# Weight splitting in an attention and MoE kernel: other tiles for the first layer, other engines for the scaling, the high and the low parts, and another instruction for the row sums

## What is computed

```python
# attention, 8 heads of 64, a window of 128 keys, a distance bias per head
attn = softmax(where(mask, q @ k.T / 8 + bias, -1e9)) @ v          # sum + 1e-9 in the softmax
# first MLP on x = attn (512 features), 2048 hidden
xn = (x - mean) / sqrt(var + 1e-6) * g_ln
x = x + relu(xn @ w_ch1) @ w_ch2
# second MLP, 1024 hidden, gated by a 3-tap convolution along the tokens
h = relu(x @ w_in)
out = (h * sigmoid(conv3(h, conv_w))) @ w_out
```

## Time and profile before

| | us |
|---|---|
| median of 3 runs | 806.03 (805.5 to 806.35) |
| the profiled execution: its own time | 807.84 |
| the profiled execution: span of its instructions | 806.0 |
| PE busy in the span | 783.7 (97%) |
| DVE, ACT, POOL busy | 520.0, 372.3, 171.9 |
| mean granted TensorE clock | 0.998 |

### The profile page before, as it was taken

One profiled execution on the slowest core, in us unless ns is written; L12 is line 12 of the kernel. 1 busy time (PEld: TensorE's weight loads), 2 busy tenths in 40 slices (PEclk: granted clock), 3 DMA queues, 4 the chain that ended last, 5 costly groups with the idle time before them and its releaser, 6 DMA issues.

```text
span 806.0 us, 17023 instructions
## 1 busy us (share of the span) xinstructions
PE 783.7 (97%) x5809; PEld 754.6 (94%) x5809; DVE 520.0 (65%) x1419; ACT 372.3 (46%) x1033; POOL 171.9 (21%) x165
## 2 busy tenths in 40 slices
PE   9989799999999999989999999999999999999998
PEld 5668789999999999989999999999998999999998
DVE  6785777873667776456777646213259888788862
ACT  6884465652346555224655522113244444444532
POOL 5677832210212121011212101111210111011100
PEclk9999999999999999999999999999999999999999
DMA  7653512211221230122123012303230202222001
GB/s 186 172 163 99 185 37 75 71 42 59 68 68 39 74 92 21 59 71 68 39 74 86 27 59 83 106 13 96 80 100 10 82 31 81 81 81 81 22 23 45
DMA packets 56494, 59.42 MB, mean 74 GB/s; under 512 B 25184, under 2 KB 43616, under 8 KB 55904
## 3 DMA queue, kind: packets, MB, share of 16 engines
q1 hardware_dynamic: 56416, 58.43, 24.5%
HBM read 44.25 MB, written 14.16 MB: 72 GB/s over the span
## 4 chain that ended last, share of the span: by engine, by line
PE 74%; issue 11%; DVE 8%; ACT 3%; POOL 3%; POOLq 0%; DVEq 0%; ACTq 0%
PE bank L1378 21%; PE bank L1380 20%; PE bank L1379 20%; PE bank L1317 3%; PE bank L1349 3%; PE bank L1331 3%; PE bank L1276 1%; PE bank L1302 1%; POOL small L684 1%; PE bank L1289 1%; DVE prob L1029 1%; ACT prob L805 1%; DVE small L1022 1%; DVE q_st L1116 1%; PE bank L1265 1%
## 5 line engine op out<-in xcount | busy, mean ns | idle before, releaser
L1378 PE MATMUL bank<-xn_hi,wa_hi 128*128 128x288 f32 x512 | 156.4, 306 | 2.7 <-issue 2.7
L1378 PE MATMUL bank<-h_hi,wb_hi 128*128 128x288 f32 x512 | 156.3, 305 | 1.1 <-DVE h_lo L1086 0.6
L1379 PE MATMUL bank<-xn_lo,wa_hi 128*128 128x288 f32 x512 | 152.1, 297 | 0.0
L1380 PE MATMUL bank<-xn_hi,wa_lo 128*128 128x288 f32 x512 | 151.8, 296 | 0.0
L1379 PE MATMUL bank<-h_lo,wb_hi 128*128 128x288 f32 x512 | 150.9, 295 | 0.0
L1380 PE MATMUL bank<-h_hi,wb_lo 128*128 128x288 f32 x512 | 150.7, 294 | 0.0
L835 ACT ACTIVATE h_hi<-bank 128x288 fp32r<-128x288 f32 x128 | 52.4, 409 | 173.1 <-PE bank L1380 172.2
L1086 DVE SCALAR_TENSOR_TENSOR h_lo<-bank,h_hi 128x288 fp32r<-128x288 f32 x128 | 58.2, 455 | 113.9 <-ACT h_hi L835 112.3
L1378 PEld LDWEIGHTS bank<-xn_hi,wa_hi 128*128 128x128 f32 x512 | 96.7, 189 | 4.2 <-issue 3.4
L1378 PEld LDWEIGHTS bank<-h_hi,wb_hi 128*128 128x128 f32 x512 | 96.5, 189 | 3.3 <-issue 2.0
L1379 PEld LDWEIGHTS bank<-xn_lo,wa_hi 128*128 128x128 f32 x512 | 96.9, 189 | 0.0
(11 more groups left out here) (132 smaller groups left out, 1679.0 us busy)
## 6 DMA issues: line engine op xcount, KB each, us to landing
k_raw<-qkT SPq DMA_DIRECT2D x48, 144.0 KB, 2.9
q_raw<-qkT SPq DMA_DIRECT2D x48, 144.0 KB, 2.9
x_in<-x_spill SPq DMA_DIRECT2D x8, 580.0 KB, 4.3
ch_in<-ch_spill SPq DMA_DIRECT2D x8, 580.0 KB, 5.2
x_spill<-xT SPq DMA_DIRECT2D x4, 1152.0 KB, 4.2
ch_spill<-ch_stage SPq DMA_DIRECT2D x32, 144.0 KB, 1.9
out<-out_stage SPq DMA_DIRECT2D x32, 144.0 KB, 1.8
wa_raw<-w SPq DMA_DIRECT2D x16, 256.0 KB, 3.7
```

Source lines behind the costliest of these rows:

```text
L1378: nc.tensor.matmul(dst, w_h, a_h, start=start, stop=False)
L1379: nc.tensor.matmul(dst, w_h, a_l, start=False, stop=False)
L1380: last = nc.tensor.matmul(dst, w_l, a_h, start=False, stop=stop)
```

## The change

For the first MLP's first layer, a tile is now 128 rows by 512 columns of `w_ch1` as it lies in memory: tile i = 4j + d has rows 128d and columns 512j. So each of its rows has one gain, which ACT takes as `scale` while it rounds, and DVE as the scalar of the one instruction that makes the low part, (raw x gain) - hi. `first_product` f now reads from the four tiles 4(f//4) + d and waits for all four. `w_gain` is gone. All tiles of `w_ch2` are rounded and subtracted on POOL. The times of the tiles are new tables, six of `wa` and nine of `wb` in the prologue. The row sums and the constant 1e-9 lie side by side (`sum_eps`), and a tensor_reduce over the pairs replaces tensor_scalar_add; in the prologue it stands at +1.4 instead of +1.78 slots. In the pass last, the tiles of the second MLP wait for the last of the four blocks that share their columns; the last four (`LATE_W` = 12) come in the second MLP's first section, rounded by ACT and subtracted by POOL.

```diff
+W1_PROLOGUE, W1_FIRST = [2.1, 3.1, 4.1, 5.1, 6.1, 7.1], [0.25, 2.05, 3.85, 5.65, 7.45, 9.25, 11.05, 12.85, 14.65, 16.45]
+W2_PROLOGUE, W2_FIRST = [3.0, 4.5, 6.0, 7.5, 9.0, 10.2, 11.4, 12.6, 13.8], [1.5, 3.9, 6.3, 8.7, 11.1, 13.5, 15.9]
...
+LATE_W = NW2 - DC
+def last_step(m):
+    return m // DC * DC + DC - 1
...
-        out += [(2 * (F1 + m) + 1, ("W", NW1 + m)) for m in range(NW2)]
+        out += [(2 * (F1 + last_step(m)) + 1 + 2 * (m % DC), ("W", NW1 + m)) for m in range(LATE_W)]
...
+                if layer == 1:
+                    j, d = divmod(i, DC)
+                    return w1[P * d:P * (d + 1), DM * j:DM * (j + 1)], wa_hi[:, i, :], wa_lo[:, i, :]
...
+        def w1_part(w, f, d):
+            return w[:, DC * (f // DC) + d, P * (f % DC):P * (f % DC + 1)]
+        def hi_by_pool(n):
+            return n < NW1 and not first_layer(n)
+        def lo_by_pool(n):
+            return not first_layer(n) if n < NW1 else n % 2 == 1 or n >= NW1 + LATE_W
...
-                nc.gpsimd.tensor_tensor(kc, kc, g_col[:].unsqueeze(2).broadcast_to((P, DC, P)), ALU.mult).then_inc(w_prep, 1)
...
+            for m in range(LATE_W, NW2):
+                w_lo(NW1 + m)
...
-                nc.scalar.activation(w_tile(n)[1], w_raw(n), ACT.Copy).then_inc(w_hi_ready, 1)
+                nc.scalar.activation(w_tile(n)[1], w_raw(n), ACT.Copy, scale=gain(n) if first_layer(n) else 1.0).then_inc(w_hi_ready, 1)
...
+                        if first and 1 <= f <= NW2 - LATE_W:
+                            w_hi(NW1 + LATE_W + f - 1)
...
-                nc.vector.tensor_scalar_add(row_inv[:, r:r + n], row_sum[:, r:r + n], SUM_EPS).then_inc(half_sum, 1)
+                nc.vector.tensor_reduce(row_inv[:, r:r + n], sum_eps[:, r:r + n, :], AX, ALU.add).then_inc(half_sum, 1)
...
+                if first_layer(n):
+                    nc.vector.scalar_tensor_tensor(lo, w_raw(n), gain(n), hi.bitcast(F32), ALU.mult, ALU.subtract).then_inc(w_split_dve, 1)
...
-("HS", 1.78, "half_inverse")
+("HS", 1.4, "half_inverse")
...
-                    wait_w_split(pe, 2 * f)
+                    wait_w_split(pe, W_ORDER.index((1, last_step(f))))
...
+            for n in (LATE_W - 2, LATE_W - 1, NW2 - 1):
+                wait_w_split(pe, NW1 + n)
```

More of the change, by code:

```diff
@@ L23 @@
 ACT = mybir.ActivationFunctionType
+AX = mybir.AxisListType.X
 P = 128
@@ L102 @@
 X_SPILL_AT, LOAD_AT = 6.5, -1.9
-W_TIMES = [2.4, 3.6, 4.8, 6.0, 7.2, 8.4, 9.2, 10.0, 10.8, 11.6, 12.4, 13.2, 14.0, 14.8]
-W_PROLOGUE = len(W_TIMES)
-W_HI_POOL = (4, 8, 12)
-W_PACE, W_AHEAD = 1.0, 6
-LEAD_GAIN_PROLOGUE = 0.5
-assert W_PROLOGUE % 2 == 0
+W1_PROLOGUE, W1_FIRST = [2.1, 3.1, 4.1, 5.1, 6.1, 7.1], [0.25, 2.05, 3.85, 5.65, 7.45, 9.25, 11.05, 12.85, 14.65, 16.45]
+W2_PROLOGUE, W2_FIRST = [3.0, 4.5, 6.0, 7.5, 9.0, 10.2, 11.4, 12.6, 13.8], [1.5, 3.9, 6.3, 8.7, 11.1, 13.5, 15.9]
+W_TIMES = sorted([(kind == "first", t, layer) for layer, kind, times in ((1, "prologue", W1_PROLOGUE), (1, "first", W1_FIRST),
+                                                                      (2, "prologue", W2_PROLOGUE), (2, "first", W2_FIRST)) for t in times])
+W_ORDER = [(layer, sum(x[2] == layer for x in W_TIMES[:n])) for n, (_, _, layer) in enumerate(W_TIMES)]
+W_AHEAD = 6
+assert len(W_ORDER) == NW1 and len(set(W_ORDER)) == NW1
 def head_items(start, slots=6.0, frame=FRAME, lag=LAG):
@@ L165, in timeline @@
         out += [(t, ("WARM", n)) for t, n in WARM]
-        out += [(t, ("W", n)) for n, t in enumerate(W_TIMES)]
+        out += [(t, ("W", n)) for n, (first, t, _) in enumerate(W_TIMES) if not first]
         return sorted(out, key=lambda x: x[0])
@@ L169, in timeline @@
     if kind == "first":
-        out += [(0.25 + W_PACE * (n - W_PROLOGUE), ("W", n)) for n in range(W_PROLOGUE, NW1)]
+        out += [(t, ("W", n)) for n, (first, t, _) in enumerate(W_TIMES) if first]
         out += HALF_FIRST
@@ L445, in w_raw @@
             if n < NW1:
-                return (wb_raw if n % 2 else wa_raw)[:, n // 2, :]
+                layer, i = W_ORDER[n]
+                return (wa_raw if layer == 1 else wb_raw)[:, i, :]
             return w_stage[:, n % NSTAGE, :]
@@ L700, in w_hi @@
             def w_hi(n):
-                if n % 2 == 0:
-                    pool.wait_ge(w_prep, n // 2 + 1)
                 wait_w_loaded(pool, n)
@@ L710, in run @@
             def run(kind, batch):
-                lead = LEAD_GAIN_PROLOGUE if kind == "prologue" else 1.5
                 early = 0.7 if kind == "prologue" else 1.0
-                delays = [("PREP", 0.1, "k_lo"), ("PREPV", 0.1, "v_lo"), ("IN", 0.5, "inv"), ("W", -lead, "w_gain"), ("W", 0.0, "w_hi"),
+                delays = [("PREP", 0.1, "k_lo"), ("PREPV", 0.1, "v_lo"), ("IN", 0.5, "inv"), ("W", 0.0, "w_hi"),
                           ("W", 0.3, "w_lo"), ("Y", 1.0, "y"), ("HS", -early, "scale"), ("HS", 0.9, "pads")]
@@ L888, in run @@
                         evacuate(batch, a[0])
-                    elif name == "w" and a[0] not in W_HI_POOL:
+                    elif name == "w" and not hi_by_pool(a[0]):
                         w_hi(*a)
@@ L1021, in normalise @@
                 dve.wait_ge(exp_ready, NT * hd + t1)
-                nc.vector.tensor_scalar_add(row_sum[0:rows, t0:t1], row_sum[0:rows, t0:t1], SUM_EPS).then_inc(sum_step, 1)
+                nc.vector.tensor_reduce(row_inv[0:rows, t0:t1], sum_eps[0:rows, t0:t1, :], AX, ALU.add).then_inc(sum_step, 1)
                 dve.wait_ge(sum_step, step + 1)
-                nc.vector.reciprocal(row_inv[0:rows, t0:t1], row_sum[0:rows, t0:t1]).then_inc(sum_step, 1)
+                nc.vector.reciprocal(row_inv[0:rows, t0:t1], row_inv[0:rows, t0:t1]).then_inc(sum_step, 1)
                 dve.wait_ge(sum_step, step + 2)
@@ L1152, in run @@
                         evacuate(batch, a[0])
-                    elif name == "w" and not by_pool(a[0]):
+                    elif name == "w" and not lo_by_pool(a[0]):
                         w_lo(*a)
```

87 lines of the change are left out of this document (40 added, 47 removed).

## The result

The changed kernel takes 807.04 us (median of 20 runs, 805.96 to 808.67) beside 805.88 for the kernel before on the same chip; the ratio is 1.0014, 95% interval 1.0008 to 1.0020. On another chip it was 807.66 us, 1.0018 (1.0009 to 1.0028). So it makes no difference of note, where 801.3 was forecast with a range up to 806.5. The profiled execution has a span of 806.3 us and took 808.14, 0.3 more than that of before.

A forecast was written before the change was run, and what follows sets the result against it. The prediction took PE as the bound, busy 783.7 of 806.0 us, with 13.5 us within reach of the weight work. Terms of 8.8 us back less 4.1 lost gave 4.7, so 801.3 us, range 796.5 to 806.5.

The forecast's parts named there:

- 10 to 61: Prologue heads and the stretch behind, in us: 0.8 back up to 45, 3.0 back from 45 to 61.
- rival 3: Slower: each low part on DVE waits for a whole POOL operation, making DVE the bound; 815.5 us, chance 0.12.
- 75 to 102: Third power, DVE chain from 90 to 98 and clock after it: 0.8, 2.1 and 1.7 us back.
- the two terms for PE's waits, 0.8 and 2.1: PE idle time won back: 0.8 us from 75 to 90, 2.1 us from 90 to 98.
- The term for the third power: 75 to 90: less weight work on POOL ahead, power 1.1 us sooner; 0.8 us back, bounds 0 and 1.8.
- three low parts ahead of the first transposed probabilities: 90 to 98: three low parts in DVE's list cost 2.1 us, against 3.2 and 1.0 us of waits removed.
- The third term: 98 to 102: PE idles less before it, so the clock stays full; 1.7 us back, bounds 0 and 1.7.
- 102 to 115: Two more low parts cost 2.1 us against 2.5 us of removed waits: 0.4 back, bounds -0.5 and 1.6.
- 115 to 594: No weight work, and later tiles in the pass last run beside a full PE: nothing won or lost.
- The second MLP: From 594: four POOL subtractions each hold DVE 1.0 us, ACT's roundings add 0.1; cost 4.1 us, bounds 0 and 6.9.
- Rival 4: All as forecast, but the clock falls in the second MLP, costing 1.7 us: 803.0 us, chance 0.08.
- Rival 2: The start wins half: power still late, low parts on the path after 84, clock falls; 806.3 us, chance 0.16.

The follow-up runs named there:

- e15: The kernel before with the reduction over pairs alone, half_inverse left at 1.78: 803.68 us, ratio 0.9955 to before.
- "after": Column of relu start times in the changed kernel's first profile, relative to the kernel before (minus is sooner); changed kernel 807.04 us.
- the second profile: The changed kernel run once more, nothing altered, for another profile: 807.66 us.
- e5: The changed kernel with POOL's seven second-layer tiles of the first pass 4.8 time units later, behind the powers: 803.97 us, ratio 0.9964 to before.
- e17: Changed kernel with second-MLP tiles all in the last pass, seven second-layer tiles and three first-layer low parts later, ACT's loop padded: 795.87 us.
- e12: The changed kernel with the addition of a constant instead of the reduction, half_inverse still at 1.4: 808.90 us, ratio 1.0038 to before.
- e8: The changed kernel with 13 matmuls by zeros added in two of PE's waits: 807.16 us, ratio 1.0009 to before.
- e9: The changed kernel with 25 more instructions on ACT ahead of its steady-pass loop: 806.26 us, ratio 0.9992 to before.

## Why the prediction was wrong

**10 to 61, forecast 3.8 won: right, and somewhat more.** 5.0 us by the first relu, 4.1 by PE's idle time in the windows. The powers come when their statistics are there (ready at 40.28, started at 40.36), the reduction takes 0.15 us, and PE lacks 0.27 us from 45 to 61. The low part takes 0.735 us at best and 0.99 on the mean of the six in the prologue, so it waits 0.25 us where 0.35 was taken, and rival 3, which decides from 0.65, never got near. But the prediction split the credit wrongly: it gave most to the power and little to the reduction, which by e15 is worth 3.6 us alone on the kernel before, passes included.

**75 to 102, forecast 0.8 + 2.1 + 1.7 = 4.6 won: this is the step that failed.** "after" stands at -4.52 at the relu before (69.98 us in the kernel before) and at -4.67 at 101.16, so nothing was won; in the second profile it was 1.1 us. What failed are the two terms for PE's waits, 0.8 and 2.1. The term for the third power counted 1.1 us sooner, and the power is that much less late after its statistics (1.57 us instead of 2.60). But PE's wait there is 1.93 us as before 1.8: DVE's own new low parts delay the statistics (1.72 us at 71.14) and lengthen POOL's operations ahead of the power. The prediction charged DVE for meeting POOL and forgot to charge POOL. And of "three low parts ahead of the first transposed probabilities", the last collided (1.39 us) right ahead of `pt_lo`, where nothing hid it; PE lacks 2.1 us from 90 to 98, not 1.2. e5, which only moves POOL's tiles behind the powers, wins 4.5 us between the same two relus, and e17, with the last low parts moved as well, 6.0.

The third term, "the clock back, 1.7", had its sign wrong in the profile: two spells instead of one. It rested on the idle time of whole stretches ("1.79 idle of 15 kept the full clock"), but in both profiles of the changed kernel a spell follows a wait of 1.9 us like those that kept the clock before, and in e12 none does. One profile of before couldn't price this term, and its bound from below should have been a second spell, not nothing. It isn't what is missing, though: e8, at full clock all through, wins 1.4 us between those relus, 0.3 more than the second profile with its one spell, and up to relu 13 it wins 2.1 of the 5.0 us that were forecast up to 115.

**102 to 115, forecast 0.4: right**, 0.7.

**115 to 594, forecast nothing: wrong by 1.3 us.** "No weight work, so nothing" overlooked that the place of a loop in the program and the phase of the engines change with what is ahead of it.

**The second MLP, forecast 4.1 lost: right**, 4.3 in the profile, by the mechanism named: four subtractions, four DVE rows longer by 0.8 to 1.1 us. Rival 4's clock fell too, 607 to 614, but PE was waiting for DVE anyway. In the first profile and in e8 the clock is low for 7 us and the loss is 4.3; in the second profile, e5 and e9 it is low for 3.4 us and the loss is 4.0, and in e12, with POOL's subtractions and no spell, 4.1. So a spell costs 0.3 us here at the most, not 1.7.

The sum of the profile is 5.3 - 1.3 - 4.3 = -0.3 instead of 8.8 - 4.1 = 4.7. Rival 2, "the start wins half", gave 806.3 and comes nearest in number and, with its low parts on the path after 84 and the clock that still falls, in kind.
